# Where the next tile's four transposes stand in TensorE's queue: between the two hidden turns of a half step, or behind both

## What is computed

```python
for e in range(E):                      # 8 experts, x is [3072, 512]
    mask = e_idx == e
    h = np.maximum(x[mask] @ w1[e], 0.0)      # w1[e]: [512, 1024]
    ye = h @ w2[e]                            # w2[e]: [1024, 512]
    out[mask] = gate_w[mask, None] * eom[mask, e, None] * ye
```

## Time and profile before

| | |
|---|---|
| three runs | 1114.06, 1116.91, 1117.62 us; median 1116.91 |
| the profiled execution | 1117.62 us, span 1116.0 us |
| PE busy | 1024.7 us, 92% of the span |
| PEld / DVE / ACT / POOL busy | 737.1 / 598.8 / 350.9 / 193.2 us |
| mean granted TensorE clock | 0.961 of full speed |
| first expert layer | about 298 to 692 us, 11 half steps |
| second expert layer | about 716 us to the end, 11 half steps |

### The profile page before, as it was taken

The page is one execution under the profiler, slowest core; times in us unless marked ns, Lnnn a source line. Parts: engine busy times, 40 slices in busy tenths (PEclk is TensorE's granted clock), DMA queues, the critical chain, the costliest instruction groups (busy, mean ns, idle before and its releaser), DMA issues.

```text
span 1116.0 us, 24722 instructions
## 1 busy us (share of the span) xinstructions
PE 1024.7 (92%) x6870; PEld 737.1 (66%) x6870; DVE 598.8 (54%) x2637; ACT 350.9 (31%) x1130; POOL 193.2 (17%) x385
## 2 busy tenths in 40 slices
PE   5999999929989999999999997399999999999994
PEld 3888888828657666766666765376566775776772
DVE  6778888833565666567656567323433243243331
ACT  3767767622222222223222122012212122122111
POOL 1122222120212121212122112101111111111111
PEclk9999999968999999999999999599999999999998
DMA  9856668350151515151505151603445151551010
GB/s 188 164 144 151 152 143 267 150 185 20 45 178 41 189 34 186 32 190 41 179 30 190 32 190 32 210 29 121 162 141 196 38 193 46 179 191 40 32 38 22
DMA packets 123417, 133.75 MB, mean 120 GB/s; under 512 B 82253, under 2 KB 82253, under 8 KB 123217
## 3 DMA queue, kind: packets, MB, share of 16 engines
q1 hardware_dynamic: 91904, 50.23, 18.3%
q10 hardware_dynamic: 24096, 62.22, 16.0%
q0 software_dynamic: 7344, 20.47, 4.9%
HBM read 105.82 MB, written 25.83 MB: 118 GB/s over the span
## 4 chain that ended last, share of the span: by engine, by line
PE 54%; issue 25%; DMA 11%; POOL 5%; DVE 3%; POOLq 1%; ACT 0%; SPq 0%; DVEq 0%; ACTq 0%
PE bank L1418 14%; PE bank L1428 13%; DMA bins<-q_in,sidx 10%; PE bank L1292 8%; PE bank L1334 4%; PE bank L1373 4%; PE bank L1459 4%; PE bank L1439 4%; POOL q_in L777 3%; POOL pad_p L725 2%; PE bank L1308 2%; PE bank L1447 1%; DMA n_words<-in_n_local_dram 0%; DMA x_g<-bins 0%; POOLq L801 0%
## 5 line engine op out<-in xcount | busy, mean ns | idle before, releaser
L1418 PEld LDWEIGHTS bank<-x_gt,w_sb 128*128 128x128 f32 x2624 | 312.3, 200 | 23.1 <-issue 20.5
L1418 PE MATMUL bank<-x_gt,w_sb 128*128 128x128 f32 x2624 | 317.5, 284 | 10.3 <-issue 8.5
L1428 PE MATMUL bank<-w_sb,h_t 128*128 128x512 f32 x656 | 288.3, 592 | 0.0
L1428 PEld LDWEIGHTS bank<-w_sb,h_t 128*128 128x128 f32 x656 | 121.4, 190 | 137.3 <-issue 137.3
L725 POOL TENSOR_TENSOR pad_p<-zeros 128x1 f32<-128x1 f32 x158 | 37.6, 238 | 854.8 <-DVE y_two L1211 272.5
L903 ACT ACTIVATE h_t<-bank 128x256 f32<-128x256 f32 x164 | 62.5, 383 | 283.8 <-PE bank L1418 272.8
L1234 DVE CUSTOM_DVE_ANT_0 v_win<-y_two,nbias 128x512 f32<-128x512 f32 x192 | 120.4, 689 | 1.4
L1206 DVE CAST sidx<-r 128x1 int32<-128x1 f32 x31 | 4.8, 154 | 147.2 <-PE bank L1428 118.1
L940 ACT ACTIVATE y_two<-y_two 128x512 f32<-128x512 f32 x32 | 20.2, 632 | 200.2 <-DVE y_two L1211 165.5
L1439 PE MATMUL bank<-w_sb,x_gt 128*64 128x256 f32 x704 | 80.7, 382 | 0.0
L1459 PE MATMUL bank<-w_sb,h_t 128*64 128x512 f32 x352 | 80.4, 598 | 0.0
(11 more groups left out here) (192 smaller groups left out, 1272.7 us busy)
## 6 DMA issues: line engine op xcount, KB each, us to landing
w_sb<-in_moe_w_dram ACTq DMA_DIRECT2D x28, 2048.0 KB, 11.8
x_g<-bins SPq DMA_DIRECT2D x130, 133.0 KB, 2.7
w_sb<-in_moe_w_dram SPq DMA_DIRECT2D x4, 2048.0 KB, 14.8
q_in<-in_q_dram SPq DMA_DIRECT2D x24, 256.0 KB, 4.0
k_in<-in_k_dram SPq DMA_DIRECT2D x24, 256.0 KB, 4.5
v_own<-in_v_dram SPq DMA_DIRECT2D x24, 256.0 KB, 3.5
v_win<-v_own SPq DMA_DIRECT2D x20, 192.0 KB, 3.3
nbias<-in_moe_expert_emb_dram ACTq DMA_DIRECT2D x1, 2048.0 KB, 9.8
```

The lines of the kernel that those rows point to most:

```text
L1418: m_ = T.matmul(banks[k][:, f * P:(f + 1) * P], w1_sb[:, w1 + c * FF + at:w1 + c * FF + at + P], x_gt[:, c, :], start=(c == 0), stop=(c == ...
L1428: m_ = T.matmul(banks[4][:, :], h_t[:, c, :], w2_sb[:, w2 + c * DM:w2 + (c + 1) * DM], start=(c == 0), stop=(c == FC - 1))
```

## The change

In the half-step loop of TensorE, the four transposes of the next tile, `x_tr(i + 1)`, no longer stand between the two hidden turns. The helper `h_turn` now issues both turns, with the wait of each ahead of it, and `x_tr(i + 1)` comes behind them, ahead of `second_half`. No instruction is added or taken out, the waits keep their values, and the other engines' programs and the full-step loop are as before.

```diff
-                def h_turn(i, k):
-
-                    pe.wait_ge(L.h, PIECES * i + (k + 1 + FIRST))
-                    for m in range(2):
-                        t_ = T.transpose(banks[2 + k][:, m * P:(m + 1) * P],
-                                         h_tok[:, (2 * k + m) * P:(2 * k + m + 1) * P], ident[:, :])
-                    t_.then_inc(L.mm1, 2)
+                def h_turn(i):
+                    for k in range(2):
+
+                        pe.wait_ge(L.h, PIECES * i + (k + 1 + FIRST))
+                        for m in range(2):
+                            t_ = T.transpose(banks[2 + k][:, m * P:(m + 1) * P],
+                                             h_tok[:, (2 * k + m) * P:(2 * k + m + 1) * P], ident[:, :])
+                        t_.then_inc(L.mm1, 2)
...
                         first_half(i, w1)
-                        h_turn(i, 0)
                         x_tr(i + 1)
-                        h_turn(i, 1)
+                        h_turn(i)
                         second_half(i, w2)
```

## The result

Six runs of the changed kernel had a median of 1123.75 us (1118.85 to 1125.09), six of the kernel before 1116.23 us (1112.74 to 1118.91). The ratio is 1.0063, with a 95% interval from 1.0036 to 1.0091: slower by 7.5 us. I had forecast 1119.3 us, given a range up to 1122.4, and put the chance of a slowdown of over 0.3% at 0.26. The profiled execution took 1119.41 us, span 1117.8, only 1.8 us more than the one before.

What follows compares the result with a forecast made beforehand. TensorE's order was taken to bound second-layer half steps, with VectorE's `hot1` covering delays in the first. 11 x 0.22 = 2.4 us plus 0, on the median of 1116.9, gave 1119.3 us; range 1115.4 to 1122.4.

Steps and rivals of the forecast that it cites:

- What bounds the kernel: Half steps: TensorE delays under 0.70 us cost nothing in the first layer; in the second layer a delay costs itself.
- `x_tr` comes behind it: Second-layer half step: `x_tr` follows the second turn without a bubble, so `second_half` can start at 792.50 instead of 792.25.
- the second turn isn't earlier: Second-layer half step: the second turn now waits for ReLU 1, loading at 791.78 to 791.82 against 791.83 before.
- The price of the order that I did price: Per half step: 0.25 us of later `second_half`, taken as 0.22 us; bounds 0.11 and 0.44 us.
- so the old wait of 0.17 us is gone: Ahead of `second_half`: copy 0 is there at 792.16, so the 0.17 us wait vanishes, saving nothing of its own.
- A gain is excluded ... copy 0, whose own start isn't touched: Second-layer half step: `second_half` can't start ahead of copy 0, whose start at ReLU 1's end stays put.
- First layer, 0 us: First-layer half steps: the same 0.22 us is hidden beside VectorE, the wait for `hot1` shrinking from 0.70 to 0.48 us.
- The loads of the next tile: Behind `x_tr`: ScalarE's copy at 793.23 and SP's loads aren't late; the last lands at 798.3, wanted at 799.73.
- Covered: Rival, second layer: loads slip ahead or ReLU 1 releases sooner, 0.11 us x 11, 1118.1 us; chance 0.14.
- fully exposed: Rival, second layer: a released queue stumbles once more, 0.44 us x 11 = 4.8, 1121.7 us; chance 0.18.
- The clock falls in the second layer: Rival: opened gaps lower the clock, 1.63 us for each of eight blocks, 1132 us; chance 0.04.
- The clock falls less often in the first layer: Rival: shorter idle before full steps avoids falls of 1.63 us each, all six giving 1109.5 us; chance 0.07.

Runs made afterwards that it cites:

- experiment 3: New order in the first layer's half steps only, old order in the second's, against the kernel before: 1113.26 us, ratio 0.9975.
- experiment 2: New order in the second layer's half steps only, old order in the first's, against the kernel before: 1119.74 us, ratio 1.0031.
- version 4: Both hidden turns ahead of `x_tr`, the order the prediction had priced, against the kernel before: 1114.64 us, ratio 0.9995.
- version 6: First turn inside `first_half` ahead of its last quarter, ScalarE making copy 0 before ReLU 1, against the kernel before: 1117.29 us, ratio 0.9995.
- experiment 1: The changed kernel run once more without edit, against the kernel before: 1116.32 us against 1115.25, ratio 1.0015.
- version 7: Old order plus three products of constants behind each expert's half steps in the first layer, against the kernel before: 1114.79 us, ratio 0.9974.
- 9: Old order plus one product of constants behind each expert's half steps in the first layer, against the kernel before: 1109.13 us, ratio 0.9925.

## Why the prediction was wrong

**What bounds the kernel: right.** A delay inside a first-layer half step costs nothing (3: no slowdown; waits 19.2 to 14.7 us, the 0.40 us being less than the 0.70 of the shortest wait) and one inside a second-layer half step costs itself (2: all of it).

**The failed step: "`x_tr` comes behind it".** Everything in "the change part by part" was worked out for an order that the diff doesn't make. It gave "the second turn isn't earlier", a wait of the turn for ReLU 1, and "copy 0 is still there". In truth the first turn is late, copy 0 with it, and `second_half` waits for copy 0. The second turn has the same six transposes ahead of it as before and starts, by its loads, within 0.01 us of where it stood behind the product. The rows of before would have given nearly the size, as an estimate. Turn 0 goes back by `x_tr`'s 0.44 us; it had ended at 791.67, so 792.11; copy 0 of 0.38 us starts 0.05 later, no longer held by ReLU 1, and ends at 792.54; `second_half` follows 0.09 behind, at 792.63 instead of 792.25: 0.38 us, 4.2 us for the layer, against 0.40 and 4.4 in the trace. It would have made the forecast 1121.1 us, and the measured median would still lie 2.6 us above it.

**The price of the order that I did price: partly right.** Run as version 4 it cost 0.34 us per half step in the trace, not 0.22. The release (0.05 us), the absence of a stumble and the turn's 0.27 us held. The term that failed is the 0.43 us from `x_tr` to the next group, taken from a full step; it measured 0.53. With it failed "so the old wait of 0.17 us is gone": this idle time lay ahead of `second_half` in versions 4 and 6 too, where no copy held it. "PE's queue had 0.17 us of room" was the same misreading. The upper bound of 0.44 held.

**"A gain is excluded ... copy 0, whose own start isn't touched": wrong for this change.** Its start is just what is touched, by 0.43 us. That the kernel came out slower, as forecast, is no merit of the reasoning: the cost came by another path.

**First layer, 0 us: right**, with 0.40 us off each wait instead of 0.22, since the delay is larger.

**The loads of the next tile: right**, not in any wait; `x_copy` still starts behind the gate's exponentials.

**Rivals.** "Covered" and "fully exposed" belonged to the other order. "The clock falls in the second layer" didn't happen: its full steps took 14.45 to 14.65 us as before. "The clock falls less often in the first layer" is at least part of where the scatter comes from; how far it went is said below.

**Why 7.5 us and not 4.4.** What could be shown: the clock's falls cost about 1.6 us each, they aren't the same from run to run (six slow full steps in the traces of before and after, four in the trace of experiment 1, which is the same kernel as after), and with the falls filled the change costs 5.3 ± 0.9 us. A line through the 35 runs of before that experiments 1 to 4 shared, the first seven of the changed kernel, and the 12 of each of these experiments against their mean granted clock, with one slope and a level for each kernel, has a slope of 0.74 us less for each 0.001 of clock more. At equal clock the levels above before are +3.9 us for experiment 1, +3.6 for experiment 2, -0.5 for experiment 3 and +2.3 for experiment 4, each with an error of about 0.45. The first three lie within two errors of the 4.4, 4.4 and 0 from the traces; experiment 4 lies three below its 3.7. For version 6, on its own chip, the same working gives +4.1 ± 0.6, and its trace 0.42 x 11 = 4.6. The changed kernel's first runs had a mean clock of 0.960, those of experiment 1 0.964, and that difference makes about 3 of the 5 us between their means. The rest, which leaves the first runs 1.7 us above experiment 1 at equal clock (error 0.7), has no cause shown.

**Does the clock fall less often in the first layer?** In experiments 1, 3, 4 and 6 `second_half` ends later there, as the faster rival supposes. Their mean clocks were 0.964 to 0.966, those of the kernel before 0.961 on either chip, and experiment 2, which leaves the first layer alone, had 0.961. The four differences are 2.6 to 7 times their own errors. At the slope above, 0.004 and 0.005 of clock are worth 3 to 4 us, which is most of what the traces of versions 4 and 6 show and their totals don't; in experiment 3 it is the 2 us by which it came out faster. Their traces have 4, 6, 4 and 3 slow full steps behind half steps, where the kernel before has 6 and experiment 2 has 5. So the later runs bear out this rival, at 2 to 4 us, where the prediction gave it a chance of 0.07. They show the higher clock, not how the order brings it about. And the changed kernel's first runs had 0.960, and 6 slow steps in their trace. Why they are the exception stays open.

## What to carry to other kernels

Write out the old and the new sequence of a diff as two lists before pricing anything: a line that the diff leaves unmarked has moved forward when the line above it is taken out. Where an engine takes its work in the written order, work that nobody awaits yet belongs behind work that starts another engine's chain: put the instruction that ScalarE waits for first and the filler into the time in which ScalarE works. Where the same kernel's runs differ by more than the effect, time the affected steps in the trace, and compare totals at equal granted clock as well.

## What the hardware showed beyond this

- Short partly idle stretches cost more than their length here: six of seven full steps behind first-layer half steps took about 9.0 us instead of 7.4, at a mean clock of 0.81. One product (three took 2.34 us in version 7) in the idle time ended all of them in its trace (9) and was worth 8.0 us in the median, more than the whole change cost.
- Changes of kind on TensorE aren't free. Ahead of `second_half` the load sat idle for 0.17 us both with copy 0 only just done and with it long done (4, 6), and a group of transposes behind matmuls took 0.15 us more than its transposes' spacing (6, and 0.37 against 0.22 us in the earlier trace rows).
- A wait put down to one engine can hide such a gap: the 1.8 us that the earlier trace rows charge to ScalarE's copy over 11 half steps were not saved in version 4, where copy 0 was long done and the same 0.17 us of PEld's idle time are charged to "issue".
